# A fused recurrence and two feed-forward layers: first-layer units of 2 to 4 chunks, second-layer units of 4, weights split in another order, row copies from two queues

## The reference, cut to what matters

```python
mag = np.sqrt(a_re * a_re + a_im * a_im)
scale = np.minimum(mag, 0.999) / (mag + 1e-06)
a_re_n, a_im_n = (a_re * scale, a_im * scale)
for t in range(S):
    new_re = ar * S_re - ai * S_im
    new_im = ar * S_im + ai * S_re
    S_re, S_im = (new_re + kv, new_im)      # kv = outer(k[t], v[t])
    y[:, :, t] = einsum('bhd,bhde->bhe', q[:, :, t], S_re)
x = y.transpose(0, 2, 1, 3).reshape(B * S, H * D)
h = x @ w_in;  g = h * np.clip(h + 3.0, 0.0, 6.0) / 6.0;  x = g @ w_out        # layer 1
h = x @ w_in2; g = np.maximum(h, 0.0) + alpha * np.minimum(h, 0.0); out = g @ w_out2   # layer 2
```

## Time and profile before

| what | value |
|---|---|
| median of three runs | 1018.17 us |
| profiled execution | 1019.44 us |
| its span | 1017.7 us |
| mean granted TensorE clock | 0.989 |
| TensorE matmul busy | 953.0 us, 94% |
| VectorE busy | 635.2 us, 62% |
| ScalarE busy | 493.2 us, 48% |
| GpSimd busy | 303.7 us, 30% |

### The profile page before, as it was taken

The page is one execution under the profiler, slowest core; times in us unless marked ns, Lnnn a source line. Parts: engine busy times, 40 slices in busy tenths (PEclk is TensorE's granted clock), DMA queues, the critical chain, the costliest instruction groups (busy, mean ns, idle before and its releaser), DMA issues.

```text
span 1017.7 us, 17923 instructions
## 1 busy us (share of the span) xinstructions
PE 953.0 (94%) x6882; PEld 937.2 (92%) x6882; DVE 635.2 (62%) x1116; ACT 493.2 (48%) x884; POOL 303.7 (30%) x291
## 2 busy tenths in 40 slices
PE   0466999999999999999999999999999999999997
PEld 0356999999999999999999999999999999999997
DVE  6887798888888878888872345534343434343432
ACT  7665777766687667767742443222222222121211
POOL 1224442222222222222222333333333333333332
PEclk9987999999999999999999999999999999999999
DMA  6742324343233333433321701010101010101000
GB/s 207 202 113 69 72 73 110 79 103 107 72 94 84 77 97 96 102 89 72 87 61 27 295 1 47 1 48 1 47 1 47 1 47 2 47 1 47 1 24 24
DMA packets 77862, 70.54 MB, mean 69 GB/s; under 512 B 32592, under 2 KB 73552, under 8 KB 77392
## 3 DMA queue, kind: packets, MB, share of 16 engines
q1 hardware_dynamic: 77456, 69.10, 24.7%
q10 hardware_dynamic: 320, 0.30, 0.1%
HBM read 40.90 MB, written 9.44 MB: 49 GB/s over the span
## 4 chain that ended last, share of the span: by engine, by line
PE 84%; DVE 4%; SPq 4%; ACT 3%; DMA 2%; issue 1%; POOL 1%; ACTq 0%; DVEq 0%
PE op L1136 13%; PE hp L1136 12%; PE hp L1137 12%; PE op L1138 12%; PE op L1137 12%; PE hp L1138 12%; PE yp L1124 3%; PE gp L1131 2%; PE gp L1103 2%; SPq L345 2%; SPq L348 2%; PE yp L1103 2%; DMA a_sb<-a_in 1%; PE tp L1112 1%; DMA st<-prod 1%
## 5 line engine op out<-in xcount | busy, mean ns | idle before, releaser
L463 POOL TENSOR_TENSOR g_lo<-gated,g_hi 128x384 fp32r<-128x384 f32 x256 | 267.3, 1044 | 636.7 <-ACT g_hi L572 636.7
L572 ACT ACTIVATE g_hi<-gated 128x384 fp32r<-128x384 f32 x256 | 132.9, 519 | 307.0 <-DVE gated L855 290.7
L851 DVE TENSOR_SCALAR gate<-hp,alpha_sb 128x384 f32<-128x384 f32 x128 | 79.1, 618 | 229.7 <-PE hp L1138 229.7
L1136 PE MATMUL op<-g_hi,wb_hi 128*128 128x384 f32 x384 | 134.5, 350 | 5.1 <-POOL g_lo L463 5.1
L1136 PE MATMUL hp<-x_hi,wa_hi 128*128 128x384 f32 x384 | 131.6, 343 | 4.2 <-POOL wa_lo L469 2.5
L1136 PE MATMUL hp<-x_hi,w2i_hi 128*128 128x384 f32 x384 | 130.2, 339 | 0.0
L1137 PE MATMUL hp<-x_lo,w2i_hi 128*128 128x384 f32 x384 | 130.1, 339 | 0.0
L1138 PE MATMUL hp<-x_hi,w2i_lo 128*128 128x384 f32 x384 | 129.7, 338 | 0.0
L1138 PE MATMUL hp<-x_hi,wa_lo 128*128 128x384 f32 x384 | 129.6, 338 | 0.0
L1137 PE MATMUL hp<-x_lo,wa_hi 128*128 128x384 f32 x384 | 129.6, 337 | 0.0
L1138 PE MATMUL op<-g_hi,wb_lo 128*128 128x384 f32 x384 | 129.4, 337 | 0.0
(11 more groups left out here) (108 smaller groups left out, 1737.6 us busy)
## 6 DMA issues: line engine op xcount, KB each, us to landing
st<-prod SPq DMA_DIRECT2D x94, 145.1 KB, 2.9
a_sb<-a_in SPq DMA_DIRECT2D x24, 288.0 KB, 4.0
qk_sb<-qk_in SPq DMA_DIRECT2D x24, 288.0 KB, 3.6
v_pad<-v_in SPq DMA_DIRECT2D x24, 192.0 KB, 3.7
x<-out_sb SPq DMA_DIRECT2D x8, 576.0 KB, 3.4
x_raw<-x SPq DMA_DIRECT2D x8, 576.0 KB, 4.5
out<-out_sb SPq DMA_DIRECT2D x8, 576.0 KB, 3.1
st<-prod SPq DMA_DIRECT2D x96, 32.2 KB, 1.9
```

The costliest lines, as they stand in the source:

```text
L463: pool.tensor_tensor(g_lo[:, at, :], gated[:, at * UT:(at + 1) * UT], g_hi[:, at, :].bitcast(F32), ALU.subtract).then_inc(glo_done, 1)
L572: act.activation(g_hi[:, at, :], gated[:, at * UT:(at + 1) * UT], ACT.Copy).then_inc(ghi_done, 1)
L851: dve.tensor_scalar(gate[:, at], hp[:, n % 2, 0:UT], 0.0, alpha_sb[:, m:m + 1], ALU.min, ALU.mult).then_inc(gate_done, 1)
L1136: pe.matmul(acc, lhs[0], rhs[0], start=start, stop=False)
```

## The change

The first layer's units hold 2, 2, 3, 3, 3, 3, 4 and 4 chunks (`SIZES`), so its matmuls have 256, 384 or 512 columns. The second layer has 6 units of 4 chunks, 512 columns. `places` spreads 4 to 6 items over a chunk's steps, now called A to F (`STEPS`). Only two chunks are done ahead of the first items, and the first 4 items (`ALONE`) run with no chunk beside them. The weight pieces are split in the order in which the items need them (`W_ORDER`), 8 before the first item and 2 beside each of the first 8 items. For chunks 0 and 1, ScalarE's queue issues two of the 12 row copies (before, for chunk 2 alone). `GRING` is 3 instead of 4. The input of layer 2 lands in the memory of `x_lo`'s buffers, and stores of `x2` are cut where units of 4 begin. The loads of SP are reordered in the start.

```diff
-CPU = 3
+CPU = 4
+SIZES = (2, 2, 3, 3, 3, 3, 4, 4)
-GRING = 4
+GRING = 3
+STEPS = {4: (0, 1, 1, 2, 3, 3), 5: (0, 1, 1, 2, 3, 4), 6: (0, 1, 1, 2, 3, 4), 8: (0, 1, 2, 3, 5, 6)}
+ALONE = 4
-W_SPLITS = {CPU: 4, CPU + 1: 4}
-W_EARLY = 2 * NWI - sum(W_SPLITS.values())
+W_ORDER = (A_BLOCKS[0] + B_BLOCKS[0:1] + A_BLOCKS[1] + B_BLOCKS[1:4] + A_BLOCKS[2] + B_BLOCKS[4:6] + A_BLOCKS[3]
+           + B_BLOCKS[6:])
+W_EARLY = 8
+W_ITEM = 2
...
 def items_of(s):
-    u, j = divmod(s, CPU)
-    return list(range((u - 1) * MT_FF + MT_FF * j // CPU, (u - 1) * MT_FF + MT_FF * (j + 1) // CPU)) if u > 0 else []
+    u = unit_of(s)
+    j = s - STARTS[u]
+    first = ALONE if u == 1 else (u - 1) * MT_FF - 1
+    count = u * MT_FF - (0 if u == U1 - 1 else 1) - first
+    return list(range(first + count * j // SIZES[u], first + count * (j + 1) // SIZES[u]))
...
             def stack(c):
...
-                for to, rows in high_stack(c, 1) + ([] if c == CPU - 1 else low_stack(c, 1)):
+                for to, rows in high_stack(c, 1) + ([] if c < FIRST else low_stack(c, 1)):
...
             load_a(2)
-            for c in range(2):
-                stack(c)
-                load_qk(c + 1)
-                load_w(6 + 2 * c)
-                load_w(7 + 2 * c)
-                load_a(c + 3)
+            stack(0)
+            load_qk(1)
+            load_a(3)
+            load_w(6)
+            stack(1)
...
             def hidden(n):
-                if n == 0:
-                    pe.wait_ge(w_lo_done, NWI)
+                if n < MT_FF:
+                    pe.wait_ge(w_lo_done, split_count(A_BLOCKS[m * P // WPC]))
...
-            for c in range(CPU):
+            for c in range(FIRST):
                 for k in range(2):
                     score(c, k)
                     turn_k(c, k)
                 outputs(c)
-                new_state(c)
-            for k in range(HSTEP):
-                hidden(k)
+                if c < FIRST - 1:
+                    new_state(c)
+            hidden(0)
+            hidden(1)
+            new_state(FIRST - 1)
+            hidden(2)
+            for n in range(ALONE):
+                first_half(n)
+                second_half(n)
```

More of the change, by code:

```diff
@@ L23 @@
 MT_FF = FF // P
-CPU = 3
+CPU = 4
 UT = CPU * CH
 UNITS = BATCH * SEQ // UT
+SIZES = (2, 2, 3, 3, 3, 3, 4, 4)
+U1 = len(SIZES)
+STARTS = [sum(SIZES[:u]) for u in range(U1 + 1)]
+FIRST = SIZES[0]
 WSZ = KT_DM * FF
@@ L67, in w2o_tiles, with unit_of, width @@
     return [k for k in ((2, 3) if m == 0 else (m + 3,)) if k < MT_FF]
+def unit_of(c):
+    return max(u for u in range(U1) if STARTS[u] <= c)
+def width(w):
+    return SIZES[w] * CH if w < U1 else UT
 def chunk_at(s):
@@ L143, in build @@
         x_hi = sb("x_hi", [P, 2, KT_DM, UT], F32R)
+        with ExitStack() as landing:
+            x_raw = sb("x_raw", [P, 2, KT_DM, UT], F32, landing)
         x_lo = sb("x_lo", [P, 2, KT_DM, UT], F32R)
@@ L485, in _ @@
                 low(k)
-            for s, pos, n, c0, c1, c2, c3 in places():
-                if n is not None:
-                    low(n + GSTEP)
-                for w in splits_at(s, pos):
+            for n in range(NT - GSTEP):
+                low(n + GSTEP)
+                for w in splits_at(n):
                     split_w(w)
-            for n in range(N1 - MT_FF, 2 * N1 - GSTEP):
-                low(n + GSTEP)
         @block.scalar
@@ L667, in _ @@
                         waves(c1)
-                if pos == 1:
+                if "B" in steps:
                     if keeps:
@@ L696, in _ @@
                         split_w2i(2 * (m - RAW_ITEMS[0]) + k)
-                if m == X2_ITEM and u + 1 - UNITS in range(UNITS):
-                    split_x2(u + 1 - UNITS)
+                if m == X2_ITEM and u + 1 - U1 in range(UNITS):
+                    split_x2(u + 1 - U1)
                 if n == N1 - 1:
@@ L953, in _ @@
                         state(c0)
-                if pos == 3 and c2 is not None:
+                if "E" in steps and c2 is not None:
                     residue(c2)
@@ L963, in _ @@
                         mags(c3)
-            for n in range(N1 - MT_FF, 2 * N1):
+            for n in range(N1 - MT_FF, NT):
                 u, m = divmod(n, MT_FF)
@@ L1191, in _ @@
                 outputs(c)
-                new_state(c)
-            for k in range(HSTEP):
-                hidden(k)
-            for s, pos, n, c0, c1, c2, c3 in places():
-                keeps = c0 is not None and not is_last(c0)
-                if pos == 0 and c0 is not None:
+                if c < FIRST - 1:
[4 more added lines that the diff above has]
+            hidden(2)
+            for n in range(ALONE):
+                first_half(n)
+                second_half(n)
+            for steps, n, c0, c1, c2, c3 in places():
+                keeps = not is_last(c0)
+                if "A" in steps:
                     score(c0, 0)
```

341 lines of the change are left out of this document (173 added, 168 removed).

## The result

The changed kernel takes 1058.9 us (median of four runs, 1056.7 to 1059.8), the kernel before 1018.35 beside it: ratio 1.0395, 95% interval 1.0377 to 1.0413. The span of the profiled execution is 1055.0 us against 1017.7. The forecast was 1025, slower by 7.2 us in the span; it is slower by 37.3. The sign is right, the size five times too small.

A forecast was written before the change was run, and what follows sets the result against it. TensorE bounds layer 2; in layer 1 the row-copy chain stands within tenths of TensorE's work. Terms +5.3 -4.6 -0.4 -0.5 +1.7 +15.3 -10.6 +1.0 = +7.2 on median 1018.2 give 1025 us; range 1007 to 1036.

The forecast's parts named there:

- the last unit alone: End of layer 1: the last unit's 288 matmuls run alone at 512 columns, 65.6 us instead of 50.26, +15.3 us.
- The first rival: Layer 1: copies don't hold the chunks, VectorE decides; 18 us off, 1007 us; chance 0.16.
- the fixed part of 13.3 ns: Every TensorE matmul: 13.3 ns beyond columns / 2.4 GHz whatever the width, so 512 columns take 226.7 ns.
- the chain's length: Layer 1: time per chunk from scores through gate, `forward`, copy issues and landing to the next scores; 20.5, 21.6, 22.7 us.
- the three stages: Layer 1: chunks 4 to 7 (-4.6 us), 16 to 20 (-0.4) and 20 to 23 (-0.5).
- a rival of 0.07: Layer 1: each of 7 copy-bound chunks begins with TensorE at the lower clock; some +16 us, 1041; chance 0.07.
- The start: Before chunk 4: its first scores come at 121.5 us, 5.3 later than before.
- ScalarE's stand: In the start: ScalarE waits for a `wb` piece, loaded at about 31.4 us, until 37 us or later.
- Layer 2: Second layer: 1701 matmuls of 512 columns take 389.9 us, 10.6 us less than before.
- The term that I gave to the width: Matmuls of 512 instead of 384 columns: 53.3 ns more each, for 128 more columns.
- The range: Whole kernel: 1007 to 1036 us, from the unbound-copies value to past the columns case of 1034.

The follow-up runs named there:

- e6: Changed kernel with 8 of the 12 row copies of each chunk left out, heads 6 and 7 computed from zeros; ratio 0.994 to the kernel before.
- e7: Changed kernel with ScalarE's queue issuing two of the twelve row copies in every chunk, not only chunks 0 and 1; ratio 1.011 to the kernel before.
- e8: Changed kernel with row copies reordered and counted on two semaphores, so the first scores wait for four of twelve; ratio 1.0052 to the kernel before.
- e2_fill: Changed kernel with useless 128-column matmuls ahead of the scores of chunks 4 to 7 and 17 to 20; ratio 1.0333 to the kernel before.
- e1_load: Changed kernel with the first piece of the second weight matrix loaded earlier, ahead of chunk 0's row copies; ratio 1.0303 to the kernel before.
- e14: Changed kernel with all layer 2 matmuls reading the weight tiles of layer 1's second matrix; ratio 1.0275 to the kernel before, layer 2 387.6 us.
- e15: Changed kernel with one unused 32-byte tile a partition allocated ahead of the attention's tiles; ratio 1.0298 to the kernel before, layer 2 389.5 us.

## Why the prediction was wrong

- **Most of the mechanism was right.** The chunks with fewer or narrower items are bound by their row copies (e6, e7, e8 by three ways), chunks 7 to 16 keep their pace, the last unit alone costs 15.6 us (forecast 15.3), 512 columns take 226.7 ns in layer 1, and no gain appears where TensorE was relieved. The first rival, copies that do not hold the chunks (1007), is refuted by the same three runs. One argument for the fixed part of 13.3 ns was weaker than it read: the transposes move 96 columns, so their 67.5 ns are 14 over only if the 128 weight columns set the time, which no run shows. The part itself came out: 120, 173.3 and 226.7 ns at 256, 384 and 512 columns in layer 1.
- **The step that failed most** is the chain's length, put at 20.5, 21.6 and 22.7 us for the three stages and measured at 22.1, 23.5 and 23.5: 14.6 us. I took TensorE's part of it from a trace in which TensorE never waited for more than 0.74 us inside layer 1 once the start was over, so at the full clock, and set the lower clock aside as a rival of 0.07 (+16 us, 1041), though the earlier trace rows showed it after 5.08 us of waiting. The waits of 3.94 and 4.36 us ahead of chunks 17 and 18 brought it too, and the lost clock lengthens the very chain that made the wait: its first part is 8.6 us instead of 6.6. e2_fill gives back 8.4 us of 12.2 in the two stages that it fills; the cause of the rest is open.
- **The start**, +7.9: ScalarE's stand was foreseen and its end put at "37 us or later", from the fastest of four landings, 5.6 us. The load was issued at 33.45, not 31.4 (three transfers of chunk 3's decays stood ahead of it on SP, from 31.68 on), and took 8 us, the median in the earlier trace rows; ScalarE went on at 41.40. Without the stand chunk 4 comes at 122.1 (e1_load), so the other costs of the start were mis-sized too: the 121.5 of the forecast had the stand in it.
- **Layer 2**, +7.4: the spacing of 384 columns was 173.3 ns in layer 1 and 175.9 in layer 2, both in the forecast. I carried the 2.6 ns over as a constant. At 512 columns the difference is 6.9 ns (397.3 us for 1701 matmuls are 233.6 each), and it belongs to where tiles lie (e14, e15), not to the columns. The term that I gave to the width, 53.3 ns for 128 columns, is right in layer 1 (173.3 to 226.7). By what rule the place acts is open.
- The range missed because start, chain and layer 2 were each bounded at a few us and not let add up: 7.9, 14.6 and 7.4, all to one side.

## What to carry to other kernels

When a resource that was covered by a hair becomes the bound, don't price the new wait alone: ask what the waiting engine's clock does, and whether its slower work lies in the same loop. Count what a consumer needs first, of a batch of small transfers, and give it an order and a semaphore of its own: here that is worth 35 us in the changed kernel, though only 2 us in the one before, where the chain was just covered. And a mean that differs by 1.5% between two stages with matmuls of the same shape is worth an experiment: here it was not noise.

## What the hardware showed that was not expected

Matmuls with the same shape, clock (1.00) and neighbours came 226.7 or 233 ns apart at 512 columns according to where tiles begin in the partition, by steps of 32 bytes; at 384 columns 173.8 or 176.5. Useless matmuls in TensorE's waits (twelve fillers in 2.8 us) shortened the kernel by 6 us, with a granted clock of 0.98 instead of 0.87. Twelve issues of a queue, 0.64 us each, cost more (7.7 us) than the landing of the last (2.0 us), and the small copies around the four that were waited for did not make these land later (2.1 us).
